# Two-layer gated network: the second layer's first tile of outputs by seven products instead of eight

## The reference

```python
kv  = einsum('bhsd,bhse->bhde', k, v)            # 4 batches, 8 heads, 576 positions, 64 wide
att = einsum('bhsd,bhde->bhse', q, kv)
x   = att / rms(att) * g_norm                    # -> 2304 tokens x 512
x   = ((x @ w_a) * (x @ w_b)) @ w_out            # layer one: 512 -> 1536 -> 512
out = (sigmoid(x @ w_gate) * (x @ w_val)) @ w_out2   # layer two, same sizes
```

## Time and profile before

| | us |
|---|---|
| median of 3 runs (lowest, highest) | 881.02 (880.62, 882.22) |
| the profiled execution: its own time | 879.22 |
| its span (first to last instruction) | 877.0 |
| TensorE busy | 862.5 (98%) |
| VectorE busy | 648.3 (74%) |
| ScalarE busy | 514.4 (59%) |

### The profile page before, as it was taken

The page is one execution under the profiler, slowest core; times in us unless marked ns, Lnnn a source line. Parts: engine busy times, 40 slices in busy tenths (PEclk is TensorE's granted clock), DMA queues, the critical chain, the costliest instruction groups (busy, mean ns, idle before and its releaser), DMA issues.

```text
span 877.0 us, 16391 instructions
## 1 busy us (share of the span) xinstructions
PE 862.5 (98%) x5844; PEld 835.5 (95%) x5844; DVE 648.3 (74%) x1272; ACT 514.4 (59%) x1044; POOL 19.4 (2%) x69
## 2 busy tenths in 40 slices
PE   6999999999999999999999999999999999999998
PEld 4889999999999999999999999988999999999998
DVE  4987788864888884768985888983787894676673
ACT  5856665554665674555675556563666584656453
POOL 1111110000000000000000000000000000000000
PEclk9999999999999999999999999999999999999999
DMA  9782258995777681445683588888646586445276
GB/s 346 246 297 77 95 184 314 318 323 183 240 213 268 200 296 58 144 168 193 201 276 122 181 293 279 280 288 288 209 163 253 181 293 171 150 139 199 94 240 195
DMA packets 99508, 189.81 MB, mean 216 GB/s; under 512 B 6884, under 2 KB 49124, under 8 KB 99428
## 3 DMA queue, kind: packets, MB, share of 16 engines
q1 hardware_dynamic: 99348, 188.71, 63.7%
q10 hardware_dynamic: 80, 0.07, 0.0%
HBM read 146.28 MB, written 42.47 MB: 215 GB/s over the span
## 4 chain that ended last, share of the span: by engine, by line
PE 94%; DMA 2%; DVE 2%; ACT 1%; SPq 1%; issue 1%; POOLq 0%; POOL 0%; DVEq 0%; ACTq 0%
PE psum L991 59%; PE psum L1077 10%; PE psum L1075 10%; PE psum L1030 5%; PE psum L1027 5%; PE psum L911 2%; DMA q_in<-in_q_dram 1%; PE psum L929 1%; PE psum L868 1%; DMA wo<-wo_dram 1%; PE psum L888 1%; SPq L597 0%; ACT kv L1163 0%; DVE t_raw L1638 0%; DVE h_parts L1654 0%
## 5 line engine op out<-in xcount | busy, mean ns | idle before, releaser
L991 PE MATMUL psum<-x_hi,w_hi 128*128 128x384 f32 x1008 | 341.6, 339 | 0.6 <-DVE h L1548 0.4
L991 PE MATMUL psum<-x_hi,w_lo 128*128 128x384 f32 x1008 | 338.4, 336 | 0.0
L991 PE MATMUL psum<-x_lo,w_hi 128*128 128x384 f32 x1008 | 337.9, 335 | 0.0
L991 PEld LDWEIGHTS psum<-x_hi,w_hi 128*128 128x128 f32 x1008 | 189.4, 188 | 5.9 <-issue 2.4
L991 PEld LDWEIGHTS psum<-x_lo,w_hi 128*128 128x128 f32 x1008 | 189.5, 188 | 2.3
L991 PEld LDWEIGHTS psum<-x_hi,w_lo 128*128 128x128 f32 x1008 | 189.3, 188 | 0.0
L1313 ACT ACTIVATE h_parts<-h 128x384 fp32r<-128x384 f32 x178 | 92.6, 523 | 78.0 <-PE psum L1077 25.6
L1608 DVE TENSOR_TENSOR w_lo<-s_raw,w_hi 128x512 fp32r<-128x512 f32 x144 | 98.6, 686 | 49.5 <-ACT w_hi L1220 49.2
L1608 DVE TENSOR_TENSOR w_lo<-w_raw,w_hi 128x512 fp32r<-128x512 f32 (+1 forms) x144 | 79.4, 552 | 71.3 <-ACT w_hi L1220 71.3
L1654 DVE TENSOR_TENSOR h_parts<-h,h_parts 128x384 fp32r<-128x384 f32 x178 | 96.7, 553 | 22.6 <-ACT h_parts L1313 22.3
L1077 PE MATMUL psum<-wo,h_parts 128*128 128x256 f32 x756 | 91.0, 283 | 0.0
(11 more groups left out here) (101 smaller groups left out, 816.3 us busy)
## 6 DMA issues: line engine op xcount, KB each, us to landing
wo<-wo_dram SPq DMA_DIRECT2D x60, 512.0 KB, 5.2
s_raw<-s_dram SPq DMA_DIRECT2D x48, 512.0 KB, 4.6
wo<-wo_sums_dram SPq DMA_DIRECT2D x48, 512.0 KB, 4.4
s_dram<-s_raw SPq DMA_DIRECT2D x24, 512.0 KB, 4.5
wo_dram<-wo SPq DMA_DIRECT2D x24, 512.0 KB, 5.2
wo_sums_dram<-h_parts SPq DMA_DIRECT2D x12, 1024.0 KB, 7.4
w_raw<-in_moe_w_a_dram SPq DMA_DIRECT2D x18, 512.0 KB, 3.5
w_raw<-in_moe_w_b_dram SPq DMA_DIRECT2D x18, 512.0 KB, 3.5
```

Source lines behind the costliest of these rows:

```text
L991: last = pe.matmul(to[:, 0:HT], w[:, u % 2, at, c, :], xx[:, i, c, :], start=(OPENS[i] and c == 0 and n_pass == 0), stop=(c == 1 and n_pas ...
```

## The change

Tile 3 is now a fast tile: `fast(tau)` is true for all but tile 0. Its outputs are made by the seven products, and nothing is woven between the products of its units any more. One additional matmul opens an accumulator bank. For that the split blocks of `w_out` of layer two and all their sums have to be in DRAM before tile 3's outputs, so their six jobs move into layer one's tiles: job 6 into tile 1, jobs 7 to 11 into tile 2, and jobs 3 to 5 stay in tile 1. A job of layer two also splits its two raw blocks (`split_wo_blocks`, 1024 columns on ScalarE and on VectorE) and spills them (`spill_wo_blocks`). The parts lie in slots of the `wo` ring, which is idle during units, so `load_wo` starts later in tiles 1 and 2. Because the sums' stage is `t_raw`, the sums of tokens for the next tile leave the units of tiles 1 to 3 and are made during the outputs, and `split_x` is spread from steps 17 to 29 over steps 21 to 39. Tile 4 no longer has jobs.

```diff
         def fast(tau):
-            return tau % TILES != 0
+            return tau > 0
...
-        SUMS_AT = ({6: 0, 8: 1, 10: 2}, {1: 3, 3: 4, 5: 5}, {}, {3: 0, 5: 1, 7: 2, 9: 3}, {1: 4, 4: 5}, {})
+        SUMS_AT = ({6: 0, 8: 1, 10: 2}, {1: 3, 3: 4, 5: 5, 7: 6}, {1: 7, 3: 8, 5: 9, 7: 10, 9: 11}, {}, {}, {})
+        TOKEN_SUMS_AT = ({10: (0,), 11: (1, 2)}, {}, {}, {}, {8: (0,), 9: (1,), 10: (2,), 11: (3,)}, {})
+        X_STEPS = {21 + 3 * i: i for i in range(7)}
...
+            def spill_wo_blocks(tau, job):
+                p = job - PAIRS
+                sp.wait_ge(wo_block_lo_ready, p + 1)
+                for odd in range(2):
+                    sp.dma_start(wo_dram[1, :, odd, :, p, :].rearrange("d p n -> p d n"),
...
+                    if k == 1 and sums_until(tau) > PAIRS:
+                        sp.wait_ge(wo_blocks_spilled, 32 * (sums_until(tau) - PAIRS))
+                    if k == 3:
+                        sp.wait_ge(wo_sums_spilled, 16 * sums_until(tau))
...
+                        if sums_until(tau) > PAIRS and SUMS_AT[tau]:
+                            for k in ({9: (0,), 10: (1, 2), 11: (3, 4)}, {9: (0,), 11: (1, 2)})[tau - 1].get(v, ()):
+                                load_wo(tau, k)
+                        elif 6 <= v < 6 + WO_RING:
                             load_wo(tau, v - 6)
...
-                    for k in range(WO_RING, FAST_STEPS // 2):
+                    for k in range(3 if tau == 2 else WO_RING, FAST_STEPS // 2):
...
+                    if tau == TILES and i == 0 and c == 0 and a == 0:
+
+                        pe.matmul(bank[OUT_BANKS[BANK_B][0]][:, :].rearrange("p (d n) -> p d n", d=2),
+                                  h_hi[:, h_slot(tau, 0), at], wo[:, slot, :, 0, :], start=True, stop=True)
...
+            def split_wo_blocks(tau, job):
+                dve.wait_ge(wo_block_hi_ready, job - PAIRS + 1)
+                dve.tensor_tensor(wo_block_parts(tau)[:, :, :, 1, :], wo_raw[:, :, :].rearrange("p o (d n) -> p o d n", d=2),
+                                  wo_block_parts(tau)[:, :, :, 0, :].bitcast(F32), ALU.subtract).then_inc(wo_block_lo_ready, 1)
...
-                    if 0 < tau < ALL_TILES - 1 and v >= 8:
-                        sum_tokens(tau + 1, v - 8)
...
+                        if 0 < tau < 4 and q + 1 in X_STEPS and X_STEPS[q + 1] in T_OF:
+                            sum_tokens(tau + 1, T_OF[X_STEPS[q + 1]] - 1)
```

More of the change, by code:

```diff
@@ L416, in wo_spills, with all_wo_spills @@
             return sum(1 for i in range(w + 1) if i % WO_RING == w % WO_RING and fresh_step(*WO_USES[i]))
-        def all_wo_spills(layer, slot):
-            return sum(1 for i, (tau, k) in enumerate(WO_USES)
-                       if i % WO_RING == slot and fresh_step(tau, k) and tau <= layer * TILES)
+        def all_wo_spills(slot):
+            return sum(1 for i, (tau, k) in enumerate(WO_USES) if i % WO_RING == slot and fresh_step(tau, k))
         W_GROUP = (slice(4, 6), slice(0, 2), slice(2, 4), slice(6, 7))
@@ L470, in wait_h_slot @@
                 wait_projected(eng, tau, q - ring)
-            elif tau and fast(tau - 1):
+            elif tau > 1:
                 wait_projected(eng, tau - 1, FAST_STEPS - H_RING + q)
@@ L549, in wo_sum_stage, with last_job, first_sum, of_blocks @@
             return x[:, 0:4, start:start + DH_OUT]
-        SUMS_AT = ({6: 0, 8: 1, 10: 2}, {1: 3, 3: 4, 5: 5}, {}, {3: 0, 5: 1, 7: 2, 9: 3}, {1: 4, 4: 5}, {})
-        def wo_sum_raw(tau, p):
+        SUMS_AT = ({6: 0, 8: 1, 10: 2}, {1: 3, 3: 4, 5: 5, 7: 6}, {1: 7, 3: 8, 5: 9, 7: 10, 9: 11}, {}, {}, {})
+        TOKEN_SUMS_AT = ({10: (0,), 11: (1, 2)}, {}, {}, {}, {8: (0,), 9: (1,), 10: (2,), 11: (3,)}, {})
+        X_STEPS = {21 + 3 * i: i for i in range(7)}
+        def last_job(tau):
+            return max(job for jobs in SUMS_AT[:tau + 1] for job in jobs.values())
+        def first_sum(tau, job):
+            return job == min(SUMS_AT[tau].values())
+        def of_blocks(job):
+            return job >= PAIRS
+        def sums_until(tau):
+            return last_job(tau) + 1
+        def wo_sum_raw(tau):
             if fast(tau):
@@ L677, in load_wo, with spill_wo_sums @@
+            def spill_wo_sums(tau, job):
+                layer, p = divmod(job, PAIRS)
+                sp.wait_ge(wo_sum_lo_ready, 2 * job + 2)
+                sp.dma_start(wo_sums_dram[layer, :, :, p, :, :].rearrange("s p n d -> p s (n d)"),
+                             wo_sum_parts(tau).rearrange("p s n d -> p s (n d)").bitcast(F32)).then_inc(wo_sums_spilled, 16)
             def load_wo(tau, k):
@@ L747, in _ @@
                 if tau:
-                    store(tau - 1, 0 if fast(tau - 1) else 1)
+                    store(tau - 1, 0)
                 for v in range(UNITS):
                     u = unit(tau, v)
-                    spill_sums(u + 1)
                     if fast(tau):
-                        if v - 1 in SUMS_AT[tau] and SUMS_AT[tau][v - 1] < PAIRS - 1:
-                            load_wo_sum_raw(tau, SUMS_AT[tau][v - 1] + 1)
+                        if v - 1 in SUMS_AT[tau]:
+                            job = SUMS_AT[tau][v - 1]
+                            if job < 2 * PAIRS - 1:
+                                load_wo_sum_raw(tau, job + 1)
+                            if of_blocks(job):
+                                spill_wo_blocks(tau, job)
                         if v - 2 in SUMS_AT[tau]:
@@ L1426, in _ @@
                     split_w(u + 1, 0)
-                    if not b_unit and v and tau and not fast(tau):
-                        split_h(tau, v - 1)
                     keep_s5(tau, v)
@@ L1468, in _ @@
                             out_drain(tau, 0)
-                        i = q - 17
-                        if tau + 1 < ALL_TILES and i % 2 == 0 and 0 <= i // 2 < 7:
-                            split_x(tau + 1, i // 2)
+                        if tau + 1 < ALL_TILES and q in X_STEPS:
+                            split_x(tau + 1, X_STEPS[q])
                     out_drain(tau, 1)
@@ L1797, in _ @@
                             split_h(tau, j - 1)
-                    else:
-                        if not b_unit and v and tau:
-                            split_h(tau, v - 1)
-                    if 0 < tau < ALL_TILES - 1 and v >= 8:
-                        sum_tokens(tau + 1, v - 8)
-                    if tau == 0 and v >= 10:
-                        for n in ((0,), (1, 2))[v - 10]:
-                            sum_tokens(1, n)
+                    for n in TOKEN_SUMS_AT[tau].get(v, ()):
+                        sum_tokens(tau + 1, n)
                     split_w(u + 1, 1)
@@ L1822, in _ @@
                     if v == UNITS - 1 and not fast(tau):
[L1823 removed]
+                        split_outs(tau, steps_split(v))
                     else:
```

192 lines of the change are left out of this document (93 added, 99 removed).

## The result

The changed kernel takes 875.32 us, median of 9 runs (874.48 to 878.8), against 881.02 for the kernel before (879.87 to 882.74, 9 runs). The ratio is 0.9949, with a 95% interval of 0.9936 to 0.9962: 3.3 to 5.6 us faster.

What follows compares the result with a forecast made beforehand. TensorE was taken as the bound, busy 862.5 of 877.0 us. Gains of 5.8 (tile 3) and 0.4 (tile 4) take the profiled 879.22 to 873.0; the median's 1.80 more gives 874.8, range 873.4 to 878.0.

Steps and rivals of the forecast that it cites:

- Tile 3, 5.8 gained: Tile 3's units and outputs: 139.20 us becomes 133.38 as direct steps and their waits give way to 256-column matmuls.
- The narrow pitch: Tile 3's new outputs: a matmul of 256 columns takes 0.120 us, against 0.229 for one of 512.
- Tile 4, 0.4: Tile 4's units: without its two jobs they shorten from 88.21 to 87.79 us, bounds 0 and 0.67.
- VectorE in tiles 1 and 2 at 0: Units of tiles 1 and 2: 4.0 us of VectorE work per added job fits; at most about 0.4 lost per job.
- The first wait of the earlier trace: VectorE in an even unit: waits of 0.52 and 0.92 us swallow the new split's 1.2.
- VectorE in tile 3 at 0: Tile 3's units: four sums of weights per unit fit, flush in even units with 0.4 us behind; bound 2.0.
- Token sums in the outputs at 0: Outputs of tiles: token sums and split_x, 3.8 us more on VectorE, fit there at no cost.
- DMA in tile 2 at 0, bound 3: Tile 2: 4.72 MB per pair of units fits the queue and the last reload is just met; up to 3 us.
- step 6: Tile 2's outputs: the last sums' spill (8.0) and reload (4.4) land 13.5 us into the last unit, just met.
- late spill: Rival, chance 0.08: step 6 of tile 2's outputs waits 1 to 3 us for the reload; 876 to 878.
- Its sign: What would show a late spill: L1113 waiting for a load of w_out six steps into tile 2's outputs.
- DMA as the bound of tile 2: Rival, chance 0.05: tile 2's weights come late behind blocks and sums; 20 us lost, 895.

Runs made afterwards that it cites:

- experiment 2: Kernel before the change, each of tile 3's 216 direct output matmuls of 512 columns made as two of 256: 881.23 us, ratio 1.0004.
- Experiment 3, second_split: Changed kernel with VectorE's split of two blocks done twice in each of layer two's six jobs: 880.34 us, ratio 0.9999.
- experiment 4, even_units: Changed kernel with tile 2's five jobs one unit earlier, in units 0, 2, 4, 6 and 8: 877.66 us, ratio 0.9962.
- experiment 1, tokens_in_units: Changed kernel with the token sums for tile 4 back in units 8 to 11 of tile 3: 877.03 us, ratio 0.9949.
- after_again: The changed kernel unedited, run and profiled once more: 875.0 us, ratio 0.993.
- second_spill: Changed kernel with each layer-two job's blocks spilled twice, the copy to DRAM that nothing reads: 881.56 us, ratio 0.9998.
- jobs_reordered: Changed kernel with layer two's jobs spread, two in tile 1 and four in tile 2, layer one's between: 877.91 us, ratio 0.9968.

## Why the prediction held

874.8 us was forecast (873.4 to 878.0), 875.32 was measured. The two main terms were right in size and in mechanism. That the number came so close is in part luck: one term put at 0 lost 1.3 to 1.8 us, and the medians stand further apart than the stages say (below). By its steps:

- **Tile 3, 5.8 gained:** 5.70 measured. Units 87.9 for 87.79, outputs with the opening matmul 45.6 for 45.59. The narrow pitch was right, and experiment 2 shows that it holds with tile 3's operands as well.
- **Tile 4, 0.4:** 0.39.
- **VectorE in tiles 1 and 2 at 0:** units 87.60 and 87.54. VectorE was busy for 76.22 (78 forecast). The new split took 1.22, and the pushed chain went as worked out. VectorE in tile 2, changed kernel:

```profile
414.09 1.22 DVE L1684 TENSOR_TENSOR wo<-wo_raw,wo 128x1024 fp32r<-128x1024 f32 x1
415.22 0.55 DVE L1825 TENSOR_TENSOR h<-psum,c_a 128x384 f32<-128x384 f32 x1
415.69 0.68 DVE L1651 TENSOR_TENSOR w_lo<-w_raw,w_hi 128x512 fp32r<-128x512 f32 x1
416.29 0.55 DVE L1701 TENSOR_TENSOR h_parts<-h,h_parts 128x384 fp32r<-128x384 f32 x1
417.24 0.69 DVE L1651 TENSOR_TENSOR w_lo<-s_raw,w_hi 128x512 fp32r<-128x512 f32 x1 [0.40 <-ACT w_hi L1256]
```

  The first wait of the earlier trace rows is gone and 0.40 is left of the second: two waits swallowed the split. Experiment 3 measured the margin behind it (0.6), experiment 4 what the other place costs (4.1). For a float32 `tensor_tensor` of N columns the Trainium skill ("VectorE: DVE Perf Modes", The TRN2 errata) gives (N + 151) / 0.96 ns, 1.22 us at N = 1024; the trace agrees.
- **VectorE in tile 3 at 0:** right; the units are 0.1 above tile 5's. It is as flush as forecast: one token sum more in an even unit opens a hole of 0.7 (experiment 1), so 0.2 us was free there, and not the 0.4 that I had.
- **Token sums in the outputs at 0:** right. Tile 1's outputs took 43.68, tile 3's 45.37 without the opening matmul, with VectorE busy for 38.4 in each.
- **DMA in tile 2 at 0, bound 3:** this is the term that was mis-sized. 1.30 was lost in the first profile, 1.8 in `after_again`. The bound held, but two steps of the working did not. First, I priced only the spill of the last *sums* (step 6) and not that of the last *blocks*, which the change lists as a wait of its own: load k = 1 waits for it. Second, I took 4.4 for a reload. With a spill of 8.0 (two of 0.5 MB, 1 MB in all) and 4.4, k = 1 would have landed at 415.8 + 12.4 = 428.2, against a need at 427.48 + 2.08 = 429.56: met. But the reloads of blocks took 4.2 to 7.3 in the kernel before; at 7.3 it would have landed at 431.1, late by 1.5. Measured: the spill had landed 7.8 behind the first issue, as priced, and the load took 6.97. It was the reload that was too cheap, not the spill. The same holds at step 6: the sums' spill landed in 6.8 where I had 8.0, the reload took 6.1 where I had 4.4, and without the hole at step 2 it would have been 0.7 late, not met. The rival "late spill" (chance 0.08) was thus right about the mechanism, though its wait of 1 to 3 us (1.3 to 1.8 in fact) came four steps earlier. (Its sign names L1113; tile 2's outputs are L1111.)
- **DMA as the bound of tile 2:** no. The engines were 81% busy at 276 GB/s, and even 319 cost the units 1.8 us only, and those by ScalarE's wait for spills and not for weights.

By stage it is 6.1 - 1.3 = 4.8 us in the first profile, and 3.1 in `after_again`. The two ratios of the same kernel give 3.3 to 5.6 and 4.6 to 7.7, which overlap around 5. The medians differ by 5.7, more than the ratio's 4.5: 875.32 lies nearer to the forecast than 873.0 + 1.8 + 1.3 = 876.1 would, and that is the spread of the runs and no merit of the sum.

**Open.** Against the mean of the two profiles of the changed kernel (668.1 from tile 1 to the end), `tokens_in_units` is 2.0 us longer, `even_units` 2.2, `second_spill` 2.7, `jobs_reordered` and `second_split` 2.9. With the mean of the two ratios (0.994), the ratios should be 0.9962, 0.9965, 0.9971, 0.9974 and 0.9973. The first two and `jobs_reordered` agree with that. `second_spill` (0.9998 [0.9984, 1.0012]) and `second_split` (0.9999 [0.9986, 1.0011]) are more than 1 us slower than their stages say; their profiled executions were 2.4 and 1.6 us faster than their own medians, so one profile of each does not tell where the rest lies. Why a w_out load was late in tile 3's outputs in `after_again` and `tokens_in_units` (0.75 and 0.53) and not in the others wasn't tried.

## What to carry to other kernels

Add up what changed by stage, between points at which the limiting engine passes from one to the next: one profiled execution can hide most of a gain of 5 us behind an opening that the change does not touch, and two profiles of one kernel differed by 1.6 us behind it. On an engine that works in order, ask where an added instruction stands and what slack follows it; the same 76 us of VectorE cost nothing in one place and 4.1 us one unit earlier. Where a buffer changes hands between a spill and a load, price the whole chain (issue, spill, load) at the slow end of the landings of that very kind of transfer, and for each such buffer, not only for the last. A hole hides the next one behind it: ask of each load whether it would be in time if the hole before it were closed.
